# Eighteen matmuls on constants in TensorE's two pauses between the experts and the feed-forward

## The chip, the cores and the metric

The program runs on 1 core of a Trainium2 chip. The metric is the device time of one launch in microseconds (us), lower is better. All arithmetic is fp32, or fp32r where a tile says so.

## The reference

Three layers run one after the other on 3072 tokens (batch 4, sequence 768) of width 384 (8 heads of 48).

```python
# 1: linear attention with decay, per head
y[t]  = r[t] @ (state + outer(u*k[t], v[t]));  state = w*state + outer(k[t], v[t])
# 2: soft mixture of experts, 8 experts of 4 slots, hidden width 1024
logits = x @ phi                              # 3072 x 32
slot_input = softmax(logits, axis=0).T @ x    # 32 x 384
slot_out = relu(slot_input @ w1[e]) @ w2[e]   # per expert
x = softmax(logits, axis=1) @ slot_out
# 3: feed-forward, width 2048
out = relu(x @ w_in)**2 @ w_out
```

## The kernel before

The kernel is written engine by engine. Each engine's instructions stand in the order in which it runs them, and semaphores tie the engines together. Attention and the gathering of the slots take the first third of the span. Then come the experts, and then the feed-forward in six groups of four 128-token tiles.

The feed-forward never forms the tokens' mixed rows of width 384. It uses that the mixture has only 32 slots: `gin` is `slot_out @ w_in` (32 rows, 2048 columns), held as a rounded part `gin_hi` and its remainder `gin_lo`, and a token's hidden row is its mixing weights times `gin`. The stretch in question, in TensorE's order:

1. L1082 multiplies `out_t` by `w_in_sb` into `wide[2]` and raises `gin_mm`. ScalarE scales and rounds it to `gin_hi` (L545), VectorE forms `gin_lo` (L773).
2. L1091 and L1092 spread the two parts to all partitions, four pairs of matmuls into the banks `spread[0..3]`. ScalarE copies spread 0 and 2 to `gin` (L550, semaphore `gin_even`), VectorE copies 1 and 3 (L778, `gin_odd`).
3. `hidden(g, f, n)`, L1098, is one 512-column matmul into `h_ps[f % 4]` for block f of 16 in group g. ScalarE then writes `relu_h` (L569) and its rounded square `act_hi` (L572). VectorE writes the exact square `act` (L796) and the remainder `act_lo` (L801). `relu_h` and `act` have two buffers, `act_hi` and `act_lo` four.
4. `output(g, f, n)`, L1120, waits for `act_hi` and `act_lo` of block f and runs 12 matmuls of 384 columns: four token tiles, each `act_hi*w_hi + act_hi*w_lo + act_lo*w_hi`. `w_hi` and `w_lo` are the same split of `w_out`.

TensorE issues `hidden(f + 2)` ahead of `output(f)`. The first two `hidden` stand before the loop, after a wait for `gin_even` 1; a wait for `gin_even` 2 and `gin_odd` 2 follows them.

The split of `w_out` is done in eight pieces of 768 columns, in the same stretch. For pieces 0 to 3 ScalarE rounds (L542) and VectorE takes the remainder (L769); these stand between the first blocks' activation work. For pieces 4 to 7 GpSimd does both, one piece after the other (L439, L441). It begins when piece 4 has landed by DMA (`w_out_in[4]`), and waits for nothing of TensorE's after `slot_out_mm`. VectorE's queue from the first block on is: `act` 0, `act_lo` 0, `w_lo` 1, `act` 1, `act_lo` 1, `w_lo` 2, `act` 2, `act_lo` 2, `w_lo` 3, `act` 3, and so on.

The PSUM banks of `wide[0]` and `wide[1]` are used again as `h_ps[0..3]`, those of `wide[2]` and `wide[3]` as `out_ps[0..3]`. `ident` is the 128x128 identity, `fold4` a 128x128 constant of ones and zeros.

Of the kernel before, what the change touches and what calls it, by code (L numbers as in the profile page):

```python
# [11 lines left out]
P = 128  # L12
# [42 lines left out]
def wait(eng, semaphore, value):  # L55

    if not isinstance(value, int) or value > 0:
        eng.wait_ge(semaphore, value)


def program(nc, rk_t, rkv_n, w_t, u, phi, w1, w2, w_in, w_out, out):
# [5 lines left out]
    def place(name, shape, dt=F32, at=None):  # L67
        words = 1
        for n in shape[1:]:
            words *= n  # L70
        start = cursor[0] if at is None else at
        handle = nc.alloc_sbuf_tensor_at(name, shape, dt, offset=start)
        end = start + (4 * words + 31) // 32 * 32
        if at is None:
            cursor[0] = end
        place.end = end
        return handle


    ident = place("ident", [P, P])  # L80
    fold4 = place("fold4", [P, P])
# [95 lines left out]
    with stack:  # L177
# [14 lines left out]
        with phase:  # L192
            wide = [phase.enter_context(nc.psum_tensor(f"wide{i}", [P, 2 * BANK], F32)) for i in range(4)]
        phase = ExitStack()
        with phase:
            h_ps = [phase.enter_context(nc.psum_tensor(f"h_ps{i}", [P, BANK], F32)) for i in range(4)]
# [618 lines left out]
        def _(pe):  # L815
# [195 lines left out]
            for k in range(KD):  # L1011
# [3 lines left out]
                             start=True, stop=True).then_inc(slot_t_mm, 1)  # L1015
# [11 lines left out]
            for g in range(GROUPS):  # L1027
                if g == GROUPS - 1:
                    pe.wait_ge(w1_last_in, 16 * KD)
                for k in range(KD):  # L1030
                    for half in range(FE // BANK):
                        cols = slice(BANK * half, BANK * (half + 1))
                        for q in range(QUADS):
# [4 lines left out]
                                                    start=(k == 0), stop=(k == KD - 1))  # L1038
# [13 lines left out]
            for g in range(GROUPS):  # L1052
# [3 lines left out]
                for k in range(KE):  # L1056
                    if g == GROUPS - 1 and k % (KE // 2) == 0:
                        pe.wait_ge(w2_half_in[k // (KE // 2)], 16 * (E - W2_X))
                    for q in range(QUADS):
                        e = QUADS * g + q  # L1060
                        last = nc.tensor.matmul(wide[g][SLOTS * q:SLOTS * q + PER, 0:DM], hid_t[:, g, k, q], w2_of(e)[:, k],
                                                start=(k == 0), stop=(k == KE - 1))
# [20 lines left out]
                                            w_in_sb[:, k, BANK * q:BANK * (q + 1)], start=(k == 0), stop=(k == KD - 1))  # L1083
            last.then_inc(gin_mm, 1)

            pe.wait_ge(sel_r_done, 1)
            pe.wait_ge(gin_hi_done, 1)
            pe.wait_ge(gin_lo_done, 1)
# [6 lines left out]
            def hidden(g, f, n):  # L1095

                wait(pe, relu_done, n - 3)
                nc.tensor.matmul(h_ps[f % 4][:, :], gin[:, P * f:P * (f + 1)], mix_t[:, bass.ds(g * B, B), :],  # L1098
                                 start=True, stop=True).then_inc(h_mm, 1)
# [27 lines left out]
            pe.wait_ge(gin_even, 1)  # L1127
            hidden(0, 0, 0)
            hidden(0, 1, 1)
            pe.wait_ge(gin_even, 2)  # L1130
            pe.wait_ge(gin_odd, 2)
            def group(g, last_group):
# [55 lines left out]
```

## Time and profile before

| | |
|---|---|
| median of 3 runs | 425.84 us (424.75, 425.84, 425.99) |
| profiled execution, own time | 427.77 us |
| its span, first to last instruction | 425.7 us |
| mean granted TensorE clock | 0.968 of full |
| TensorE matmul busy | 378.1 us, 89% of the span |
| VectorE, ScalarE, GpSimd busy | 262.5, 182.0, 58.0 us |

The span is 2.07 us shorter than the profiled execution's own time, and that time is 1.93 us above the median of the runs. The profile puts the end of TensorE's L1082 at 184.44 us and the first `output` matmul at 192.17 us. A granted clock of 1.00 is 2.4 GHz and 0.50 is 1.2 GHz. One fp32 matmul call whose operands are both fp32 leaves two records in the trace (the six calls of L1073 are 12 records); one on fp32r operands leaves one.

### The profile page before, as it was taken

What the parts mean: (1) busy time and instruction counts of PE and PEld (TensorE: products, weight loads), DVE (VectorE), ACT (ScalarE), POOL (GpSimd) and SP (SyncE); (2) the same over time, 40 slices, a digit from 0 to 9 for tenths busy, and PEclk for the clock granted to TensorE, in tenths of its full rate; (3) what the DMA queues carried; (4) which work ended last, traced back from release to release, by engine and by line L of the source; (5) the groups of instructions that cost most, each with busy time, mean ns of one, the idle gap of its engine ahead of it and who ended that gap; (6) DMA issues with size and microseconds to landing.
All of it is one profiled execution on the core that took longest, in us unless ns stands there. A gap on an engine that the chain in (4) does not pass through costs nothing.

```text
span 425.7 us, 11855 instructions
## 1 busy us (share of the span) xinstructions
PE 378.1 (89%) x4840; PEld 334.1 (78%) x4840; DVE 262.5 (62%) x420; ACT 182.0 (43%) x312; POOL 58.0 (14%) x83
## 2 busy tenths in 40 slices
PE   0387889977889889878999999999999999999997
PEld 0277688775878333437999999999999999999996
DVE  7375568887876371149765756665565666566653
ACT  3012335242434210264555554645464555556552
POOL 3222132433321011038000000000000000000000
PEclk9998999998999899985999999999999999999999
DMA  6998799999992999970000200100020001002002
GB/s 154 261 249 240 216 260 266 256 254 246 257 235 86 355 372 375 406 269 0 2 1 2 74 2 0 53 22 0 0 74 0 0 31 42 0 0 74 0 2 74
DMA packets 28599, 55.43 MB, mean 130 GB/s; under 512 B 3360, under 2 KB 22816, under 8 KB 28192
## 3 DMA queue, kind: packets, MB, share of 16 engines
q1 hardware_dynamic: 28576, 55.11, 44.7%
q8 instruction: 16, 0.26, 0.3%
q14 instruction: 7, 0.06, 0.1%
HBM read 50.38 MB, written 4.72 MB: 129 GB/s over the span
## 4 chain that ended last, share of the span: by engine, by line
PE 76%; issue 11%; DMA 4%; SPq 2%; POOL 2%; DVE 2%; ACT 1%; DVEq 0%; POOLq 0%; ACTq 0%
PE out_ps L1120 49%; PE h_ps L1098 5%; PE score_ps L844 4%; PE y_ps L864 4%; DMA w_w<-in_w 3%; PE y_ps L882 3%; PE inc_ps L855 2%; PE x_ps L833 2%; DMA rk<-in_rk_t 2%; POOL state_a L406 2%; PE wide L1036 1%; PE wide L988 1%; SPq L344 1%; PE lg_ps L819 1%; PE lg_ps L826 1%
## 5 line engine op out<-in xcount | busy, mean ns | idle before, releaser
L1120 PE MATMUL out_ps<-w_hi,act_hi 128*128 128x384 f32 x384 | 131.2, 342 | 3.5 <-DVE act_lo L801 1.7
L1120 PE MATMUL out_ps<-w_hi,act_lo 128*128 128x384 f32 x384 | 131.6, 343 | 0.0
L1120 PE MATMUL out_ps<-w_lo,act_hi 128*128 128x384 f32 x384 | 131.4, 342 | 0.0
L796 DVE TENSOR_TENSOR act<-relu_h 128x512 f32<-128x512 f32 x96 | 68.8, 717 | 78.0 <-ACT relu_h L569 78.0
L569 ACT ACTIVATE relu_h<-h_ps 128x512 f32<-128x512 f32 x96 | 57.4, 598 | 101.1 <-PE h_ps L1098 101.1
L1120 PEld LDWEIGHTS out_ps<-w_hi,act_hi 128*128 128x128 f32 x384 | 73.2, 191 | 4.9 <-issue 2.9
L1120 PEld LDWEIGHTS out_ps<-w_lo,act_hi 128*128 128x128 f32 x384 | 73.4, 191 | 3.8
L1120 PEld LDWEIGHTS out_ps<-w_hi,act_lo 128*128 128x128 f32 x384 | 73.1, 190 | 0.0
L801 DVE TENSOR_TENSOR act_lo<-act,act_hi 128x512 fp32r<-128x512 f32 x96 | 68.4, 712 | 4.9 <-ACT act_hi L572 1.0
L572 ACT ACTIVATE act_hi<-relu_h 128x512 fp32r<-128x512 f32 x96 | 60.9, 634 | 3.9
L460 ACT ACTIVATE x_t<-y_ps 112x512 f32<-112x512 f32 x24 | 14.3, 598 | 77.1 <-PE y_ps L882 77.1
L1098 PE MATMUL h_ps<-mix_t,gin 128*128 (+1 forms) x96 | 38.6, 404 | 0.0
L393 POOL TENSOR_TENSOR keys_n<-keys_in,kn_pow 128x384 f32<-128x384 f32 x24 | 26.8, 1120 | 50.5 <-DMA keys_in<-in_rkv_n 35.0
L864 PE MATMUL y_ps<-queries,state_b 48*48 48x64 f32 x384 | 26.7, 226 | 3.9 <-issue 3.8
L844 PE MATMUL score_ps<-queries,keys 48*64 48x128 f32 x768 | 29.7, 289 | 0.0
L844 PEld LDWEIGHTS score_ps<-queries,keys 48*64 48x64 f32 x768 | 23.6, 142 | 5.0 <-issue 5.0
L855 PE MATMUL inc_ps<-values,keys_n 64*48 64x48 f32 x768 | 15.9, 221 | 12.3 <-DVE state_next L678 6.9
L864 PEld LDWEIGHTS y_ps<-queries,state_b 48*48 48x48 f32 x384 | 23.1, 127 | 4.5 <-issue 4.5
L657 DVE TENSOR_TENSOR scores<-score_ps,ident_sub 128x512 f32<-128x512 f32 x24 | 16.5, 689 | 16.2 <-PE score_ps L844 16.1
L855 PEld LDWEIGHTS inc_ps<-values,keys_n 64*48 64x48 f32 x768 | 13.1, 133 | 16.3 <-issue 14.8
L864 PE MATMUL y_ps<-queries,state_a 48*48 48x64 f32 x336 | 24.0, 220 | 1.7 <-issue 1.5
L642 DVE TENSOR_TENSOR keys<-rk,k_pow 112x512 f32<-112x512 f32 x24 | 16.5, 686 | 13.5 <-DMA rk<-in_rk_t 13.4
(145 smaller groups left out, 391.7 us busy)
## 6 DMA issues: line engine op xcount, KB each, us to landing
w_sb<-in_w SPq DMA_DIRECT2D x21, 512.0 KB, 7.8
rk<-in_rk_t SPq DMA_DIRECT2D x48, 192.0 KB, 7.8
w_room<-in_w SPq DMA_DIRECT2D x4, 1536.0 KB, 12.9
keys_in<-in_rkv_n SPq DMA_DIRECT2D x24, 192.0 KB, 7.9
values<-in_rkv_n SPq DMA_DIRECT2D x24, 192.0 KB, 7.1
out_dram<-y_sb SPq DMA_DIRECT2D x5, 768.0 KB, 3.5
w_x<-in_w SPq DMA_DIRECT2D x2, 1536.0 KB, 13.6
w_w<-in_w SPq DMA_DIRECT2D x4, 768.0 KB, 12.0
```

The costliest lines, as they stand in the source:

```text
L393: nc.gpsimd.tensor_tensor(keys_n[n % 2][:, :, :], keys_in[n % K_BUFS][:, :, :], kn_pow[:, hp].rearrange("p h d -> p (h d)").unsqueeze(1).b ...
L569: nc.scalar.activation(relu_h[f % 2][:, :], h_ps[f % 4][:, :], ACT.Relu).then_inc(relu_done, 1)
L572: nc.scalar.activation(act_hi[f % 4][:, :], relu_h[f % 2][:, :], ACT.Square).then_inc(act_hi_done, 1)
L642: nc.vector.tensor_tensor(keys[n % 2][0:PAIR].rearrange("p b (s t) -> p (b s) t", t=SUB), rk[n % RK_BUFS][0:PAIR, 1].rearrange("p b (s t) ...
L657: nc.vector.tensor_tensor(scores[n % 2][:, :, :, :], blocks[:, :, :, 1], ident_sub[:, :].unsqueeze(1).unsqueeze(1).broadcast_to([P, 2, B, ...
L796: nc.vector.tensor_tensor(act[f % 2][:, :], relu_h[f % 2][:, :], relu_h[f % 2][:, :], ALU.mult).then_inc(act_done, 1)
L801: nc.vector.tensor_tensor(act_lo[f % 4][:, :], act[f % 2][:, :], act_hi[f % 4][:, :].bitcast(F32), ALU.subtract).then_inc(act_lo_done, 1)
L844: last = nc.tensor.matmul(score_ps[part, at:at + P], keys[hp % 2][rows, b, part], queries[hp][rows, b, s].rearrange("p k t -> p (k t)"), s ...
L855: last = nc.tensor.matmul(inc_ps[rows, at:at + D], keys_n[hp % 2][part, b, D * h:D * (h + 1)], values[hp][part, b, D * h:D * (h + 1)], sta ...
L864: return nc.tensor.matmul(y_ps[rows, at:at + SUB], state[rows, hp, b], queries[hp][rows, b, s, 0], start=(b == 0), stop=False, skip_group_ ...
L1098: nc.tensor.matmul(h_ps[f % 4][:, :], gin[:, P * f:P * (f + 1)], mix_t[:, bass.ds(g * B, B), :], start=True, stop=True).then_inc(h_mm, 1)
L1120: last = nc.tensor.matmul(out_ps[t][:, 0:DM], a[f % 4][:, tok], w[:, f], start=(f == 0 and i == 0), stop=(f == NF - 1 and i == 2))
```

## The change

A helper `keep_awake(count, bank)` issues `count` fp32 matmuls of 128 columns, each with `ident` as one operand and `fold4` as the other, into the first 128 columns of a bank. Nobody reads the product. Seven go to `wide[0]` between L1082 and the waits ahead of L1091. Eleven go to `h_ps[2]` behind the first two `hidden` and ahead of the wait for the rest of `gin`; `h_ps[2]` is overwritten by `hidden(0, 2, 2)` afterwards. No semaphore and no other engine's program is changed.

```diff
             last.then_inc(gin_mm, 1)
 
+            def keep_awake(count, bank):
+
+                for i in range(count):
+                    nc.tensor.matmul(bank[:, 0:P], ident[:, :], fold4[:, :], start=True, stop=True)
+
+            keep_awake(7, wide[0])
             pe.wait_ge(sel_r_done, 1)
             pe.wait_ge(gin_hi_done, 1)
...
             pe.wait_ge(gin_even, 1)
             hidden(0, 0, 0)
             hidden(0, 1, 1)
+            keep_awake(11, h_ps[2])
             pe.wait_ge(gin_even, 2)
             pe.wait_ge(gin_odd, 2)
             def group(g, last_group):
```

## Rows read from the trace of the kernel before

**Rows 1.** Busy time in stretches of the span: PE, PEld, DVE, ACT, POOL, PEclk, DMA.
```profile
143.00:144.00 1.00, 0.83 (x8) 0.39 (x12) 0.97 (x3) 0.12 (x1) 0.00 (x0) 0.62 1.07 373
146.00:147.00 1.00, 1.00 (x9) 0.32 (x12) 0.57 (x3) 0.06 (x1) 0.00 (x0) 0.67 1.07 376
185.00:190.00 5.00, 3.72 (x11) 2.52 (x11) 3.13 (x5) 2.80 (x6) 2.35 (x2) 0.76 0.76 266
195.00:200.00 5.00, 3.60 (x12) 3.02 (x11) 4.97 (x4) 1.29 (x3) 4.84 (x4) 0.50 0.00 0
200.00:205.00 5.00, 4.58 (x22) 4.21 (x21) 4.93 (x6) 1.23 (x2) 1.21 (x1) 0.87 0.00 0
```
**Rows 2.** Chain that ended last, 165 to 215: start us, us, what.
```profile
178.37 1.57 PE wide L1073 x12
179.94 1.75 PE wide L1047 x16
181.69 2.76 PE wide L1082 x24
...
186.26 0.47 PE wide L1091
186.73 0.23 PE wide L1092
...
188.42 0.43 PE wide L1092
188.85 0.44 PE h_ps L1098
...
192.17 4.18 PE out_ps L1120 x12
196.35 0.44 PE h_ps L1098
...
198.18 3.75 PE out_ps L1120 x12
201.93 0.23 PE h_ps L1098
202.16 0.42 issue
202.58 2.35 PE out_ps L1120 x12
...
205.16 2.12 PE out_ps L1120 x12
```
**Rows 3.** VectorE in order of time, 184 to 206.
```profile
188.88 0.69 DVE L778 CAST gin<-wide 128x512 fp32r<-128x512 f32 x1 [0.73 <-PE wide L1092]
189.94 0.90 DVE L796 TENSOR_TENSOR act<-relu_h 128x512 f32<-128x512 f32 x1 [0.36 <-ACT relu_h L569]
190.88 1.19 DVE L801 TENSOR_TENSOR act_lo<-act,act_hi 128x512 fp32r<-128x512 f32 x1
...
195.84 2.19 DVE L801 TENSOR_TENSOR act_lo<-act,act_hi 128x512 fp32r<-128x512 f32 x1
...
199.45 2.31 DVE L796 TENSOR_TENSOR act<-relu_h 128x512 f32<-128x512 f32 x1
201.79 0.69 DVE L801 TENSOR_TENSOR act_lo<-act,act_hi 128x512 fp32r<-128x512 f32 x1
```
**Rows 4.** GpSimd in order of time, 187 to 206.
```profile
187.57 0.82 POOL L439 CAST w_hi<-w_out_sb 128x768 fp32r<-128x768 f32 x1 [24.43 <-DMA w_out_sb<-in_w_out]
188.47 1.82 POOL L441 TENSOR_TENSOR w_lo<-w_out_sb,w_hi 128x768 fp32r<-128x768 f32 x1
190.24 1.29 POOL L439 CAST w_hi<-w_out_sb 128x768 fp32r<-128x768 f32 x1
...
198.79 2.41 POOL L441 TENSOR_TENSOR w_lo<-w_out_sb,w_hi 128x768 fp32r<-128x768 f32 x1
```
**Rows 5.** Groups of instructions by shape, PE, 176 to 186: busy us, mean ns.
```profile
L1073 PE MATMUL wide<-pick,hid 128*128 128x128 f32 x12 | 1.6, 284 | 0.0
```

## The prediction

> **What bounds the kernel now.** I read the busy times by stretch first. The clock column is 0.76 over 185 to 190, 0.50 over 195 to 200 and 0.87 over 200 to 205 [rows 1]. If it changes once in each of the outer stretches, it fell after 2.6 of 5 us, at 187.6, and rose 1.3 us into 200 to 205, at 201.3: 13.7 us at 1.2 GHz. It fell shortly after the pause between L1082, which ends at 184.45, and L1091 at 186.26 [rows 2]. The change evidently addresses that.
>
> Then I read the chain of waits for what the slow clock costs. Twelve `output` matmuls take 4.18 us in the slow stretch, 2.35 us at 202.58 behind a wait and 2.12 us at 205.16 behind none; a `hidden` costs 0.44 against 0.23 [rows 2]. That chain looks as if TensorE set the time all the way. But TensorE also stands still, from 189.3 to 192.17 apart from one more `hidden`, from 196.79 to 198.18, and from 202.16 to 202.58 [rows 2]. What ends these waits decides what a faster TensorE is worth.
>
> So I went to VectorE and GpSimd in order of time. `act_lo` 0 ends at 190.88 + 1.19 = 192.07, `act_lo` 1 at 195.84 + 2.19 = 198.03, `act_lo` 2 at 201.79 + 0.69 = 202.48 [rows 3]. `output` 0, 1 and 2 start 0.10, 0.15 and 0.10 us later. The profile names `act_hi` for the second, but that is block 3's; `output(0, 1, 1)` waits for block 1's parts. All three are VectorE's.
>
> Why is VectorE late? A 512-column operation takes it 0.69 us alone (201.79), but 0.90, 1.19, 2.19 and 2.31 us while GpSimd works [rows 3]. The ends tell how. GpSimd's L441 ends at 188.47 + 1.82 = 190.29 and `act` 0 at 190.84, 0.55 later. L439 ends at 190.24 + 1.29 = 191.53, 0.69 after `act` 0, and `act_lo` 0 ends at 192.07, 0.54 after that. The last L441 ends at 201.20 and `act` 2 at 201.76, 0.56 later [rows 3, 4]. So the two take turns, one instruction each, and each waits for the whole of the other's. The `gin` cast at 188.88, which reads PSUM, took 0.69 us in the midst of L441 and waited for nobody [rows 3, 4].
>
> The Trainium skill, "SBUF — State Buffer", section "SBUF: two separate sides", states this rule: VectorE with two SBUF inputs and GpSimd exclude each other for a whole instruction. By that rule, the trace agrees (2.31 us for a 0.69 us operation), and the sum below would be the same.
>
> What anchors the alternation is GpSimd's start at 187.57, ended by the DMA of `w_out` [rows 4]. No TensorE instruction touched by the change stands ahead of that DMA. The end of `act_lo` 2, 202.48, is fixed by it, and from `output` 2 at 202.58 TensorE runs densely to the end.
>
> **First part: seven matmuls.** The nearest rows are L1073's, also fp32, 128x128 by 128 columns, two records a call: 12 records in 1.57 us, 0.131 us each [rows 2]. Seven calls are 14 records, 1.83 us, from 184.45 to 186.28, against a start of L1091 at 186.26. Bounds: 0.109 us a record by the 16 transposes in 1.75 us [rows 2] gives 1.5 us and no delay. With no overlap at all, at 284 ns a record [rows 5], it is 3.98 us and L1091 starts at 188.43, 2.2 us late. I take 0.131, the same form. Cost about 0. If they keep the clock up, the spreads take 0.47 + 7 x 0.23 = 2.08 us and end at 188.34 rather than 188.85, and `hidden` 0 at 188.57 rather than 189.29, 0.72 us earlier.
>
> What does that buy? `relu_h` 0 would end near 189.2, and `act` 0 could be asked for then instead of at 189.94. But GpSimd's L441 runs until 190.29 [rows 4]. `act` 0 still ends at 190.84 and `act_lo` 0 at 192.07. Gain: 0. The same slack covers small delays: `act` 0 may be asked for as late as 190.24, when GpSimd's next turn is requested, 0.3 us later than before and 1.0 later than with the fast clock.
>
> **Second part: eleven matmuls.** 22 records, 2.88 us (2.4 by the transposes, 6.25 without overlap). At the fast clock `hidden` 1 ends at 188.80, the fillers at 191.68 and `hidden` 2 at 191.91, ahead of 192.17. So `output` 0 starts on time. Queued behind the fillers is `hidden` 2, which ScalarE needs only after its `w_hi` roundings and blocks 0 and 1. At 6.25 us `hidden` 2 ends near 195.3 and `output` 0 is 3.1 us late. But then `output` 0 and 1 run without a pause, 2 x (2.12 + 0.23) = 4.7 us with their `hidden`, to 200.0, still ahead of 202.48 (2.12 from the row at 205.16). Cost 0 at either bound while the clock is fast.
>
> **The rest, with the fast clock.** `output` 0 ends at 194.3 instead of 196.35 and `hidden` 3 at 194.5 instead of 196.79. TensorE then stands for 3.6 us, because `act_lo` 1 comes at 198.03 as before. In such a pause I expect the clock to fall after all, since it fell after 1.8 us here. Fast or slow, `output` 1 with `hidden` 4 takes 2.4 to 4.0 us from 198.18 and is done by 202.16, before `act_lo` 2. `output` 2 starts at 202.58. The 2.0 + 1.6 us that the two `output` may save and the 0.7 us ahead of them all become waiting. Sum: +0 us on the span of 425.7; the profiled execution would again take 427.8 and the median **425.8 us**.
>
> **Rivals.** (a) *The clock sets this stage.* If VectorE's chain moved with TensorE, everything up to 202.58 would shrink: 0.72, then 4.62 - 2.35 = 2.27, then 3.98 - 2.35 = 1.63 (12 matmuls and a `hidden`, run on without a break), sum 4.6 us, 421.2 us. For it: the chain of waits charges these matmuls. Against it: the ends of VectorE's operations, to 0.02 us. A milder form, in which VectorE only gets 0.72 us earlier, gives 425.1 and is inside no change. The Trainium skill, "TensorE: Matmul & The Clock Gate", section "Why this matters for your kernels", advises to avoid idle gaps so that throughput does not drop; by that rule alone the change gains these 4.6 us, and no row here shows it.
>
> (b) *The clock is low at the wrong time.* Before, the clock has risen by 201.3, ahead of the dense part. A clock that falls after the new 3.6 us pause could fall behind 198.18 (it fell 1.3 us after TensorE had resumed at 186.26), with `output` 1 done early and another pause of 1 to 2 us before 202.58. It would then rise later. A slow stretch at 143 to 147 lasted from 143.24 to 146.66 [rows 1], 3.4 us. Each us of it behind 202.58 costs 1 - 2.35/4.62 = 0.49 us: 3.4 us cost 1.7, 427.5 us. It decides once the rise comes 2.6 us behind 202.58 (1.28 us lost). For it: the longer pause. Against it: `output` 1 keeps TensorE busy from 198.18 as before.
>
> (c) *The fillers overrun.* If they don't hold the clock, the spreads and two `hidden` run as before to 189.73, and 22 records at twice 0.131 end at 195.5. `hidden` 2, `output` 0, `hidden` 3, `output` 1, `hidden` 4 at 1.2 GHz: 0.44 + 4.18 + 0.44 + 3.75 + 0.44 = 9.3 us, to 204.8, 2.2 us behind 202.58: 428.0 us. TensorE is then busy without a break, and in the trace the clock rose after 3.1 us of that, so this is capped; I'd expect most of it not to be paid.
>
> (d) *The fillers are too few to hold the clock, but hidden.* Then all stays as before, 425.8: no change too.
>
> **Numbers.** Forecast, clock held or not but VectorE and GpSimd decide: 0.79 (with d). (a) in full or in good part: 0.07. (b): 0.10. (c): 0.04. What a measurement can tell here is 0.3%, 1.28 us, and the three runs themselves span 1.24 us. Same gets 0.79. Faster 0.07, slower 0.14. The range takes in the scatter of the runs (424.75), the mild form of (a), and most of (b): 424.6 to 427.2.
>
> **What would show it.** The clock stays 1.00 from 184 to beyond 192. `output` 0's twelve take about 2.1 us after 192.1. VectorE's `act`/`act_lo` and GpSimd's L439/L441 keep their times to 0.1 us relative to the landing of `w_out`. The wait before `output` 1 grows from 1.4 to about 3.6 us, and `output` 2 starts 15.0 us after GpSimd's first L439, as before. The prediction is wrong if `act_lo` 2 ends earlier than 14.9 us after GpSimd's start, if `output` 2 starts later than `act_lo` 2's end plus 0.1, or if the clock is 0.50 anywhere in the dense part.

## The result, and the profile after

| | before | with the change |
|---|---|---|
| median of 6 runs, first comparison | 425.91 us (421.45 to 435.51) | 429.16 us (428.37 to 431.39) |
| ratio, 95% interval | | 1.0114 (1.0059 to 1.0170) |
| span of the profiled execution | 425.7 us | 426.4 us |
| all runs of this study, mean (number, standard deviation) | 427.81 us (123, 3.98) | 427.40 us (36, 3.42) |

Each ratio in this document leaves out executions over 1.5% above the fastest of the same kernel, a limit that lies in the midst of the scatter and so moves with the luck of the fastest one (it takes away two of the six before and none of the six with the change, and all six against all six give 1.0047), while the means of the last line keep all. 429.16 us lies outside the predicted 424.6 to 427.2. Over all runs the change differs from the kernel before by -0.42 us, with a 95% interval of 1.32 us to either side (1.96 times the root of 3.98²/123 + 3.42²/36): no change that can be seen. Taken apart by comparison, each against all runs of the kernel before beside it, the difference is +2.0, +0.8, -2.9 and +0.5 us. The medians of the two pools are 427.2 and 427.1 us. Both readings need an explanation.

The two profiled executions first. The chain of waits of the changed kernel (start us, us, what; L1089 are the fillers, L1097, L1098, L1104 and L1126 are L1091, L1092, L1098 and L1120 of before), beside [rows 2]:

```profile
182.93 1.76 PE wide L1089 x14
184.69 0.10 issue
184.79 0.47 PE wide L1097
...
186.88 0.24 PE h_ps L1104
...
187.78 1.55 DVE act L796
189.33 0.02 issue
189.35 0.99 DVE act_lo L801
...
194.34 2.19 DVE act_lo L801
196.53 0.14 issue
196.66 3.22 PE out_ps L1126 x12
199.88 0.43 PE h_ps L1104
200.31 0.76 issue
201.07 3.96 PE out_ps L1126 x12
205.03 0.23 PE h_ps L1104
205.27 2.12 PE out_ps L1126 x12
```

The reader is to see three things. The seven fillers end before `gin_lo` is ready, so L1097 is not late. The chain now runs over VectorE from 187.78 to 196.53: this is what was under the slow matmuls of before. And the slow twelve are now those of `output` 1 (in part) and of `output` 2.

VectorE and GpSimd in order of time in the changed kernel, beside [rows 3, 4]:

```profile
187.78 1.54 DVE L796 TENSOR_TENSOR act<-relu_h 128x512 f32<-128x512 f32 x1 [0.17 <-ACT relu_h L569]
189.35 1.20 DVE L801 TENSOR_TENSOR act_lo<-act,act_hi 128x512 fp32r<-128x512 f32 x1
...
197.94 2.31 DVE L796 TENSOR_TENSOR act<-relu_h 128x512 f32<-128x512 f32 x1
200.28 0.69 DVE L801 TENSOR_TENSOR act_lo<-act,act_hi 128x512 fp32r<-128x512 f32 x1
```
```profile
186.03 0.83 POOL L439 CAST w_hi<-w_out_sb 128x768 fp32r<-128x768 f32 x1 [23.29 <-DMA w_out_sb<-in_w_out]
186.94 1.83 POOL L441 TENSOR_TENSOR w_lo<-w_out_sb,w_hi 128x768 fp32r<-128x768 f32 x1
```

`act` 0 was asked for 1.75 us behind GpSimd's start instead of 2.37 (189.94 - 187.57), and it ended at 189.32, 3.29 us behind it; before it was 3.27. It took 1.54 us instead of 0.90. All that the faster clock won ahead of it, VectorE spent waiting for GpSimd's L441. `act_lo` 2 ends at 200.97, 14.94 us behind GpSimd's start; before 14.91.

The stretches of the changed kernel, same columns as [rows 1]:

```profile
190.00:195.00 5.00, 2.62 (x14) 2.24 (x13) 4.96 (x4) 3.48 (x6) 4.84 (x4) 1.00 0.00 0
195.00:200.00 5.00, 3.34 (x13) 3.06 (x13) 5.00 (x3) 0.63 (x1) 4.62 (x3) 0.78 0.00 0
200.00:205.00 5.00, 4.24 (x14) 3.96 (x14) 4.40 (x7) 1.23 (x2) 0.00 (x0) 0.54 0.01 3
```

The clock was held through both pauses. It fell at 197.8 (0.78 over 195 to 200), after TensorE had stood from 193.2 to 196.66, and rose at 204.6. So 3.6 us of the dense part, from `output` 2 at 201.07 on, ran at 1.2 GHz. The sum of the span: GpSimd's start moved from 187.57 to 186.03 (-1.54), `output` 3 starts 19.24 us behind it instead of 17.59 (+1.65), and `output` 3 to the end takes 221.13 us instead of 220.53 (+0.60). That is +0.71, and the spans differ by 0.70. Whether the +1.65 and the +0.60 belong to the change is what the experiments had to tell.

### The profile page after: what moved, and what is told of

Its sections match the earlier page's. It is cut to its first block, busy times and chain, and to the rows that moved or that the text cites. A ratio compares the mean times of both kernels' runs of the same rounds, so it can differ in the third digit from the quotient of the medians.

```text
span 426.4 us, 11927 instructions
## 1 busy us (share of the span) xinstructions
PE 380.6 (89%) x4876; PEld 337.3 (79%) x4876; DVE 263.3 (62%) x420; ACT 182.2 (43%) x312; POOL 56.9 (13%) x83
## 4 chain that ended last, share of the span: by engine, by line
PE 72%; issue 12%; DMA 6%; DVE 3%; SPq 3%; POOL 2%; ACT 1%; DVEq 0%; POOLq 0%
PE out_ps L1126 48%; PE h_ps L1104 5%; PE score_ps L844 3%; DMA w_w<-in_w 3%; PE y_ps L864 3%; PE y_ps L882 2%; DMA keys_in<-in_rkv_n 2%; POOL state_a L406 2%; DMA rk<-in_rk_t 2%; PE inc_ps L855 1%; PE wide L988 1%; PE wide L1036 1%; PE x_ps L833 1%; SPq L317 1%; PE lg_ps L826 1%
## 5 line engine op out<-in xcount | busy, mean ns | idle before, releaser
L1126 PE MATMUL out_ps<-w_hi,act_hi 128*128 128x384 f32 x384 | 131.4, 342 | 4.8 <-DVE act_lo L801 3.4
L1126 PE MATMUL out_ps<-w_lo,act_hi 128*128 128x384 f32 x384 | 131.1, 341 | 0.0
L1126 PE MATMUL out_ps<-w_hi,act_lo 128*128 128x384 f32 x384 | 130.9, 341 | 0.0
L1126 PEld LDWEIGHTS out_ps<-w_hi,act_hi 128*128 128x128 f32 x384 | 72.6, 189 | 6.0 <-ACT act_hi L572 4.7
L1126 PEld LDWEIGHTS out_ps<-w_lo,act_hi 128*128 128x128 f32 x384 | 73.0, 190 | 4.3
L1126 PEld LDWEIGHTS out_ps<-w_hi,act_lo 128*128 128x128 f32 x384 | 72.9, 190 | 0.0
L1104 PE MATMUL h_ps<-mix_t,gin 128*128 (+1 forms) x96 | 38.2, 400 | 0.0
L393 POOL TENSOR_TENSOR keys_n<-keys_in,kn_pow 128x384 f32<-128x384 f32 x24 | 25.4, 1060 | 50.6 <-DMA keys_in<-in_rkv_n 38.0
L844 PE MATMUL score_ps<-queries,keys 48*64 48x128 f32 x768 | 30.8, 298 | 0.0
L844 PEld LDWEIGHTS score_ps<-queries,keys 48*64 48x64 f32 x768 | 24.6, 148 | 4.8 <-issue 4.8
L642 DVE TENSOR_TENSOR keys<-rk,k_pow 112x512 f32<-112x512 f32 x24 | 17.4, 726 | 11.4 <-DMA rk<-in_rk_t 11.3
```

What stands on the lines that cost most here:

```text
L393: nc.gpsimd.tensor_tensor(keys_n[n % 2][:, :, :], keys_in[n % K_BUFS][:, :, :], kn_pow[:, hp].rearrange("p h d -> p (h d)").unsqueeze(1).b ...
L642: nc.vector.tensor_tensor(keys[n % 2][0:PAIR].rearrange("p b (s t) -> p (b s) t", t=SUB), rk[n % RK_BUFS][0:PAIR, 1].rearrange("p b (s t) ...
L844: last = nc.tensor.matmul(score_ps[part, at:at + P], keys[hp % 2][rows, b, part], queries[hp][rows, b, s].rearrange("p k t -> p (k t)"), s ...
L1126: last = nc.tensor.matmul(out_ps[t][:, 0:DM], a[f % 4][:, tok], w[:, f], start=(f == 0 and i == 0), stop=(f == NF - 1 and i == 2))
```

## The experiments

**The change again, and the kernel before against itself.** Runs of the kernel before that lie 14 us apart leave open what a ratio is worth. So both kernels were timed three times more, the kernel before as if it were a change.

> The change once more, beside the kernel before on the same chip. Theory A (VectorE and GpSimd taking turns fix the start of output 2 at 15.0 us behind GpSimd's first L439; the fillers only move the 1.2 GHz stretch into the dense part): output 2 at +15.0, the twelve matmuls of output 2 slow, 1 to 2 us lost, ratio 1.002 to 1.005. Theory B (the 1.1% measured is not all this: part of it is scatter between executions of attention and the transfers, which the change does not touch): the ratio differs from 1.011 by more than its interval, and the spans scatter by more than 1 us for both kernels. Theory C (the fillers slow something directly, all 3.2 us): ratio 1.007 to 1.011 again, with the loss inside 180 to 206 us.

> The kernel before, unchanged, timed against itself: a ratio of 1 within its interval. It shows how far the spans of one kernel scatter, and at which clock each ran. Theory A with B: the scatter is 1 us or more, and goes with where the clock rises around output 2.

> The change a third time. Theory B (the 1.1% first measured is scatter): output 2 at +15.0, output 3 between +17.6 and +19.2, and a ratio that by itself tells no more than the kernel before against itself did (1.013). Theory C: a ratio of 1.01 or more, and larger than that of the unchanged kernel in the same call.

> The kernel before, unchanged, once more against itself, as the measure of what such a ratio is worth. Theory B: its ratio and that of the change beside it overlap. Output 2 at +15.0; output 3 at +17.6 or +19.2, by where the clock rises.

> The change a fourth time, for the scatter. By the positions read so far it costs 0.6 us by its block time and, by where the clock rises, nothing to 1.6 us that the kernel before pays too in part of its executions: pooled over all runs the two differ by 0 to 2 us. If the 1.1% first measured were the change's, the pooled difference would be 3 to 5 us here and over all.

> The kernel before against itself a third time, in the same call as the change. A ratio off 1 by up to 1.3%, as the first two were (1.013 and 0.993), if executions drift in the course of a call. Output 2 at +15.0, block time 2.3467.

Read from the profile of each: GpSimd's first L439, and how long after it `output` 2 and 3 start. "Block" is the mean distance of two blocks in the dense part.

| kernel | ratio (95%) | ratio of the means of all runs | L439 at, us | output 2 | output 3 | block, us |
|---|---|---|---|---|---|---|
| before, first profile | | | 187.57 | +15.01 | +17.59 | 2.3467 |
| before, second | 1.0127 (1.0045 to 1.0209) | 1.0051 | 185.17 | +14.99 | +19.18 | 2.3467 |
| before, third | 0.9933 (0.9893 to 0.9972) | 0.9974 | 180.69 | +15.01 | +17.60 | 2.3467 |
| before, fourth | 1.0009 (0.9965 to 1.0054) | 1.0015 | 185.48 | +15.02 | +17.61 | 2.3533 |
| change, first profile | 1.0114 (1.0059 to 1.0170) | 1.0047 | 186.03 | +15.04 | +19.24 | 2.3533 |
| change, second | 1.0068 (0.9982 to 1.0155) | 1.0019 | 181.81 | +15.03 | +17.63 | 2.3533 |
| change, third | 0.9918 (0.9876 to 0.9959) | 0.9924 | 188.89 | +15.03 | +19.31 | 2.3533 |
| change, fourth | 0.9969 (0.9909 to 1.0029) | 1.0016 | 186.94 | +15.03 | +17.65 | 2.3533 |

The unchanged kernel gave 1.013 against itself, with an interval that excludes 1, and 0.993 with one that excludes it on the other side. So such an interval is too narrow here: executions of one kernel scatter by 4 us, and the few of one comparison are no fair draw of them. The first 1.011 is of this size. Theory B holds. Theory C, which wanted 3.2 us, falls by the -0.42 us over all runs.

The table also settles the two terms. `output` 2 starts at +15.0 in all eight. `output` 3 comes either at about +17.6 or at about +19.2, by where the clock rises, and both kernels do both. The expectation that the twelve of `output` 2 would be slow in the change came true in two of its four profiles. Here is the kernel before in its second profile, chain of waits:

```profile
195.76 3.25 PE out_ps L1120 x12
...
200.16 3.95 PE out_ps L1120 x12
```

Its `output` 2 at 200.16 took 3.95 us, as slow as that of the change in its first profile. And in the change's second profile it is fast:

```profile
192.42 3.89 PE out_ps L1126 x12
...
196.84 2.36 PE out_ps L1126 x12
```

The three new profiles of the kernel before show one thing more. Counted from L439, the clock first fell at +0.05 us in the first profile, but at +4.9, +4.1 and +4.2 in the others, in or just behind the next pause. The pause that the seven fillers fill left it alone there. In the second profile the spreads take 0.23 us each with no filler, and `act` 0 waits for GpSimd just as it does in the change:

```profile
185.72 0.23 PE wide L1092
185.95 0.24 PE h_ps L1098
...
186.85 1.60 DVE act L796
```

So the 0.72 us that the prediction expected the fillers to win ahead of `act` 0 are there in most executions without them.

**One filler group alone.**

```diff
-            keep_awake(11, h_ps[2])     # first run
-            keep_awake(7, wide[0])      # second run
```

> Only the seven matmuls ahead of L1091. Theory A: L1091 waits for gin_lo as before, output 2 still starts 15.0 us behind GpSimd's first L439. The clock holds past 187 us and falls in one of the two later pauses (2.9 and 3.6 us, TensorE nearly idle); if it falls in the first of them, output 1 runs slow and it rises by output 2, loss under 0.5 us; if in the second, as with both, the loss is 1 to 2 us. Theory C: a cost in proportion to the fillers, 7 of 18, so about 1.2 us.

> Only the eleven behind the first two hidden. Theory A: the clock falls near 187.6 as in the kernel before, the eleven run at 1.2 GHz in part (up to 5.8 us), TensorE is then busy long enough for it to rise before output 0 or in it; the 3.6 us pause follows and the clock falls again; output 2 at +15.0 unless the eleven end past +8. Loss 0 to 2 us. Theory C: 11 of 18, about 2 us, at any phase.

First seven: ratio 1.0031 (0.9951 to 1.0111), `output` 2 at +15.03, `output` 3 at +17.62. The clock held through the first pause. It fell at 186.3, in the pause ahead of `output` 0 that the eleven would have filled, and rose at 196.5, ahead of `output` 2, with `output` 1 slow (3.95 us) and nothing lost. That is the first of the two cases expected; it came before the 187 us named there because everything lies 5.2 us earlier in this execution (L439 at 182.38). Second eleven: 1.0148 (1.0065 to 1.0231), of the size of the unchanged kernel's 1.0127. `output` 2 at +15.03, `output` 3 at +18.95. Here I had expected a fall at 187 for want of the seven, and it did not come: the clock was 1.00 until 201.3. It fell under `output` 2 instead and rose at 204.7:

```profile
196.09 2.36 PE out_ps L1125 x12
198.44 0.23 PE h_ps L1103
198.68 1.83 issue
200.51 3.50 PE out_ps L1125 x12
```

Whether the first pause lowers the clock is thus not decided by the fillers in it; three of the four profiles of the kernel before, with none, held it there as well. The cost in proportion to the fillers that theory C wanted does not show.

**The later pauses filled too.**

```diff
                     elif not last_group:
                         hidden(g + 1, f + 2 - NF, n + 2)
+                    if isinstance(g, int) and g == 0 and f == 1:
+                        keep_awake(13, h_ps[0])
                     output(g, f, n)
```

The second run of these has seven more, into `h_ps[1]`, at f == 2.

> The change plus thirteen more matmuls of the same kind into h_ps[0] ahead of output 1, in the pause of 3.4 us that TensorE has there. Theory A: the clock stays at 2.4 GHz from attention to the end, output 2 starts at +15.0 and takes 2.35 us; against the change 1.7 us are won back, against the kernel before 0 to 1 us faster, ratio 0.998 to 1.0. Theory C: 31 fillers cost more than 18, ratio 1.015 or more. If VectorE moved with TensorE (the prediction's rival a), 4 us faster than before.

> As the run with thirteen more, and seven more again ahead of output 2 (into h_ps[1]), in the pause of about 1.8 us that is left there. Theory A: no pause of TensorE over 1 us is left behind attention, the clock is 2.4 GHz from about 150 us to the end; output 2 starts 15.0 us behind GpSimd's first L439 and output 3 17.6 us behind it, the least seen so far. Against a kernel whose output 3 starts at +19.2 that is 1.6 us, and nothing against one at +17.6. The total scatters by more than that.

With thirteen: ratio 1.0126 (1.0050 to 1.0201), `output` 2 at +15.05. The expectation missed: the clock held through the 3.4 us pause, but fell at 201.8, 0.6 us behind the next one, of 1.83 us, and `output` 3 came at +19.14. With seven more the chain of waits reads

```profile
191.43 2.36 PE out_ps L1126 x12
...
195.84 2.36 PE out_ps L1126 x12
198.43 2.12 PE out_ps L1126 x12
```

and the stretches from 150 to 400 us

```profile
150.00:205.00 55.00, 50.23 (x412) 34.95 (x405) 27.85 (x32) 19.86 (x33) 15.00 (x13) 1.00 0.61 223
205.00:400.00 195.00, 195.00 (x1082) 191.43 (x1081) 119.25 (x177) 106.09 (x176) 0.00 (x0) 1.00 0.06 21
```

TensorE stays at 2.4 GHz in both, and `output` 2 still starts at +15.04 (GpSimd's L439 at 180.80), `output` 3 at +17.63. This is the cleanest test of the prediction's sum: with the slow stretch gone, nothing ahead of `output` 2 is won. The ratio was 0.9928 (0.9876 to 0.9979); the unchanged kernel's in the same comparison was 0.9933. The mean of its 12 runs is 427.3 us.

**Thirty-one instead of eleven.**

> Thirty-one instead of eleven behind the first two hidden, 38 calls in all, as many as in the run with seven more ahead of output 2, but all ahead of the loop. It asks two things. Overrun: 62 records at 0.119 us are 7.4 us from about GpSimd's start + 1.2, so output 0 starts 4 us late, near +8.9, and output 0 and 1 run on to about +13.6 at 2.4 GHz: by theory A output 2 still starts at +15.0. Block time of the dense part, 2.3467 us in the kernel before and 2.3533 in the change: if it goes by how many instructions stand ahead of the loop it is 2.3467 here, as in the other kernel with 38 calls; if it goes by something that fillers in these two places cause, 2.3533.

```profile
187.48 6.92 PE h_ps L1089 x62
194.40 0.23 PE h_ps L1104
194.63 2.12 PE out_ps L1126 x12
...
199.38 1.84 issue
201.21 2.35 PE out_ps L1126 x12
```

`output` 0 starts at +8.47 (L439 at 186.16), some 4 us late, and `output` 2 at +15.05. That is how much slack TensorE has in this stage: 20 calls too many move nothing behind `output` 1. This kernel was executed once (426.32 us), so only positions are read.

**GpSimd taken out of the stage.** The split of pieces 4 to 7 is done by ScalarE and VectorE, one piece behind every second block.

```diff
-            for i in range(EARLY, PIECES):          # GpSimd: the whole loop goes
...
-                    if first and f < EARLY - 1:     # ScalarE, and VectorE with rest_of_w_out
-                        round_w_out(f + 1)
+                    if first and f % 2 == 0 and f // 2 < PIECES - 1:
+                        round_w_out(f // 2 + 1)
...
+                    pe.wait_ge(w_lo_done, i + 1)    # TensorE, for all eight pieces
```

> The kernel before with GpSimd's part of the split of w_out taken over by ScalarE (rounding) and VectorE (remainder), one piece behind every second block of group 0, no fillers. Theory A: without the turns each of VectorE's operations takes its 0.69 or 0.95 us; act_lo 2 then ends some 6 us earlier (8 operations, about 6.2 us of own time from 189.9, instead of 12.6), TensorE becomes the bound from output 0 or 1 on, and the total falls by 3 to 6 us, ratio 0.986 to 0.993; how much of it depends on how long the clock stays at 1.2 GHz. Rival (the turns are off the path, the slow clock alone sets the stage): no change or slower, since VectorE gets more work.

> The same with the eighteen fillers. Theory A: now the clock matters, for nothing but TensorE sets the pace behind output 0: if the fillers hold it, output 0 to 2 run at 2.4 GHz without a long pause and this is the fastest of all, 1 to 4 us ahead of the one without fillers and 5 to 8 us ahead of the kernel before. Rival: fillers cost by themselves, then it is slower than the one without.

Without fillers: median 421.89 against 426.39 us, ratio 0.9813 (0.9756 to 0.9870), 12 and 23 runs with means of 420.4 and 427.3. The gain is larger than the 3 to 6 us expected. VectorE in order of time:

```profile
184.14 0.69 DVE L787 TENSOR_TENSOR act<-relu_h 128x512 f32<-128x512 f32 x1 [0.17 <-ACT relu_h L560]
184.88 0.69 DVE L792 TENSOR_TENSOR act_lo<-act,act_hi 128x512 fp32r<-128x512 f32 x1
185.54 0.96 DVE L760 TENSOR_TENSOR w_lo<-w_out_sb,w_hi 128x768 fp32r<-128x768 f32 x1
186.41 0.68 DVE L787 TENSOR_TENSOR act<-relu_h 128x512 f32<-128x512 f32 x1
187.13 0.69 DVE L792 TENSOR_TENSOR act_lo<-act,act_hi 128x512 fp32r<-128x512 f32 x1
```

Every operation is back at its time alone, so the 0.90 to 2.31 us of [rows 3] were GpSimd's doing. TensorE's chain is then unbroken:

```profile
185.67 2.35 PE out_ps L1108 x12
188.02 0.23 PE h_ps L1089
188.26 2.12 PE out_ps L1108 x12
```

Counted from `gin_lo`'s start (180.13), `output` 3 at 192.96 comes at +12.83; in the kernel before it comes at +19.91 (205.16 - 185.25). Those 7.1 us are the gain (7.0 to 8.7 against the four profiles of the kernel before), and the difference of the means is 6.9, give or take 3.0. The clock stayed at 2.4 GHz from 150 to 400 us with no filler at all; the long pauses are gone. The clock alone is not the gain, since the run with all four pauses filled had it too and won nothing ahead of `output` 2.

With the eighteen fillers as well: ratio 0.9865 (0.9814 to 0.9916), mean of 12 runs 421.6 us. The expectation of 1 to 4 us on top missed. The fillers now end behind `act_lo` 0 (187.11 + 0.69 = 187.80) and stand on the path:

```profile
185.95 2.45 PE h_ps L1080 x22
188.41 0.23 PE h_ps L1095
188.64 2.12 PE out_ps L1114 x12
```

`output` 3 at 195.70 comes 13.32 us behind `gin_lo`'s start at 182.38, 0.5 us later than without them. This is read from one profile of each; the two means differ by 1.2 us, less than their scatter can tell.

**The block time.** The first profiles gave 2.3467 us a block before and 2.3533 with the change, for instance (89 blocks apart)

```profile
205.27 2.12 PE out_ps L1126 x12
...
414.71 2.12 PE out_ps L1126 x12
```

that is 209.44/89 = 2.353. Over the 93 blocks behind `output` 2 it makes 0.6 us. I took it for an effect of the longer program.

> The eighteen matmuls moved behind the last output, so that nothing stands in the two pauses and the loop lies where it lay before. Block time 2.3467 if the slower one comes from fillers ahead of the loop, 2.3533 if the mere presence of a program that is longer by 18 calls does it. Output 2 at +15.0; output 3 at +17.6 or +19.2.

> Thirty-eight calls behind the last output. If the block time goes by how many calls the program holds in all, wherever they are, it is 2.3467 as in the two other kernels with 38; if 38 ahead of the loop mattered, 2.3533 or either. The end moves out by about 4.5 us for the fillers themselves.

> A single call behind the last output. Block time 2.3533 if any call makes the blocks slow, 2.3467 if one is too few to shift what decides it.

Fillers behind the last output: 2.3533 with 1, with 18 and with 38 of them; ahead of the dense part 2.3533 with 7, 11, 18 and 31, and 2.3467 in two kernels with 38 and in the one without GpSimd and without fillers. The count does not order this. The fourth profile of the unchanged kernel then showed 2.3533 too, so it is not the change's alone: it takes one of two values from one profile to another. The kernel before had the lower one in three profiles of four. The eighteen fillers in their two places had it in none of five (one of them without GpSimd's part), so a leaning is not excluded. What sets it stays open. The three kernels with fillers behind the end were executed once each (429.19 us with 18, 438.16 with 38, 425.22 with 1), and those fillers lengthen the span themselves, so only positions are read. `output` 2 was at +15.02 with 38 behind the end and +15.03 with 1, and `output` 3 at +19.32 and +19.25, late without a filler in any pause. With 18 it was at +15.21, because there the clock stayed at 1.2 GHz from 191.5 to 201.7 and `output` 1 with its `hidden` ended just too late: the one case of sixteen in which the slow clock itself moved `output` 2, by 0.2 us.

## Why the prediction was right and where it was wrong

**Right: what fixes `output` 2.** The prediction had the end of `act_lo` 2 fixed by GpSimd's start, and so by a DMA. Predicted 15.0 us behind the first L439; measured 14.99 to 15.05 in all sixteen profiles with that stage but the one at +15.21, with no filler to 38, whether the clock fell in this stretch or not. Taking GpSimd out moved it from 17.33 us behind `gin_lo`'s start (202.58 - 185.25) to 10.48 (190.61 - 180.13). The Trainium skill, "SBUF — State Buffer", section "SBUF: two separate sides", says that VectorE with two SBUF inputs and GpSimd exclude each other for a whole instruction. These runs agree: 0.69 us with GpSimd's part gone, 0.90 to 2.31 us while it works.

**Right: the two filler costs.** 1.76 us measured against 1.83 for the seven, 22 records in 2.62 us (11 calls) against 2.88, both hidden. The tolerance to an overrun, put at 6.25 us for the eleven, is shown by 31 calls in 6.92.

**Right: the pause grows.** It grew from 1.4 to 3.4 us, forecast 3.6, and the clock fell after it.

**One execution read as the rule.** The prediction took the fall at 187.6, behind the first pause, for what the kernel does. Three of four profiles of the kernel before have it 4 us later, so the seven fillers mostly guard a pause that needs no guard. It changes nothing in the sum, which gave them no gain.

**Rival (b) came true, but in both kernels, in three of the eight profiles.** In the first profile of the change the clock fell at 197.8, 1.2 us after TensorE had resumed, and rose 3.6 us into the dense part; the cost was 1.65 us where 1.7 was priced. I gave it 0.10, priced it at 427.5, outside my own range, and reckoned it as something that the change brings. The kernel before does it as well (+19.18 in one profile of four, +19.24 and +19.31 in two of four with the change), and so do the two kernels with 1 and 38 fillers behind the end. It is also the last of the prediction's signs of being wrong, a clock of 0.50 in the dense part; that sign can't tell the two kernels apart. The step "from `output` 2 at 202.58 TensorE runs densely to the end" had read one execution of the kernel before as if its clock always rose in time.

**Wrong: what a measurement can tell.** The step that failed is in "Numbers": "What a measurement can tell here is 0.3%, 1.28 us, and the three runs themselves span 1.24 us." Three runs of 424.75 to 425.99 were taken for the scatter. The 123 runs of the same kernel lie between 419.4 and 437.0 us, with a standard deviation of 4.0. Most of it comes from ahead of the changed stage: GpSimd's first L439, which a DMA releases, lies between 180.7 and 187.6 us in four profiles of one kernel, while from there to the end of the span it is 238.1 to 239.7 us. The range of 424.6 to 427.2 was therefore too narrow for any version, the unchanged one included: the latter gave medians of 429.0, 428.7 and 426.9 us when timed as a change, two of three outside. That six executions with the change gave 429.16 is mostly the draw, and a median inside the range would have been luck in the same measure. The forecast itself, no change, agrees with 36 against 123 runs to within 1.3 us (0.3%).

**Not settled: a cost below 1.3 us.** Two finer readings lean to one. The slower block time, if it belongs to the fillers, costs 0.6 us. And the time of an execution less its span was at most 2.13 us in the 117 executions of the kernel before whose span is on record, but 2.3 to 2.9 us in 14 of the 36 with the change: 0.26 us more on average, 0.46 in the first comparison. The prediction's sum went by the span and had no term for this. No experiment tells where it comes from.

**Rival (a) falls.** It wanted 4.6 us for a clock held up. The run with all four pauses filled held it, and nothing moved ahead of `output` 2. The Trainium skill, "TensorE: Matmul & The Clock Gate", section "Why this matters for your kernels", advises to avoid idle gaps so that throughput does not drop. The run with all four pauses filled agrees as to the clock (1.00 from 150 to 400 us), but here it won nothing ahead of `output` 2, because another engine ended that wait.

## What to carry to other kernels

Before you speed up or warm up an engine, look at what ends its next wait: here three `output` blocks waited for VectorE, which waited in turns for GpSimd, and moving GpSimd's work away gained 7 us where 18 or 38 fillers gained nothing. Place fillers only where a pause is sure to remain, since once the real cause was removed they stood on the path and cost 0.5 us there. Time the unchanged kernel as if it were a change before you believe an interval: three close runs say little of the scatter. Put the means of all runs beside any ratio that leaves some out. Do not take where a clock falls in one profile for what the kernel does. Positions relative to an event just ahead of the change (here GpSimd's first L439) told to 0.05 us what totals could not tell to 1.

## What was not expected of the hardware

- The 1.2 GHz stretch comes at other places in executions of one kernel: from 187.6 to 201.3 us in one, from 190.1 to 193.5 and 196.9 to 203.7 in another. A pause of 1.83 us brought it in one run (thirteen more fillers) and none in another (thirty-one instead of eleven).
- A block of 13 matmuls takes 2.3467 or 2.3533 us throughout an execution, at the same granted clock.
- A filler record of 128 columns took 0.112 us in the run of 62, less than the 0.131 of L1073 and close to the transposes' 0.109.
